# Where a fused attention and mixture kernel adds up, inverts and turns its softmax rows: moving three steps in VectorE's order of work

## The reference

```python
# stage 1: linear attention, then an MLP with a residual
q_s = softmax(q, axis=-1); k_s = softmax(k, axis=tokens)
x = q_s @ (k_s.T @ v)                                # per head
x = x + relu(normalize(x) * g_ln @ w_ch1) @ w_ch2    # normalize over 512 values
# stage 2: four causal attention experts, of which each token keeps the best two
logits = x @ w_gate                       # the two largest of 4, softmaxed, are the gates
for e in range(4):
    q, k, v = x @ wq[e], x @ wk[e], x @ wv[e]
    a = softmax(causal(q @ k.T / 8))
    out += gate_e * (a @ v @ wo[e])
```

## Time and profile before

| | |
|---|---|
| profiled execution, its own time | 1260.09 us |
| span of its trace | 1258.3 us |
| PE busy | 1229.3 us (98%) |
| DVE busy | 667.9 us (53%) |
| ACT busy | 379.5 us (30%) |
| POOL busy | 224.2 us (18%) |
| mean granted TensorE clock | 0.993 |
| stage 2 | about 891 to 1258 us, 42.4 us a batch |

### The profile page before, as it was taken

How to read it: one execution, slowest core, us unless ns; L and a number is a source line. 1 busy time by engine, 2 the same in 40 slices (tenths; PEclk the granted TensorE clock), 3 DMA queues, 4 the chain that set the end, 5 groups by cost and what they waited for, 6 DMA issues and landing times.

```text
span 1258.3 us, 19440 instructions
## 1 busy us (share of the span) xinstructions
PE 1229.3 (98%) x7136; PEld 1018.5 (81%) x7136; DVE 667.9 (53%) x1750; ACT 379.5 (30%) x858; POOL 224.2 (18%) x252
## 2 busy tenths in 40 slices
PE   8989999999999999999999999999989999999988
PEld 7878888888888888888888888888877787878876
DVE  5685365365365365365365313311576666666562
ACT  4462131131131131131131101121334445454445
POOL 3532000000000000000000000001474356445322
PEclk9999999999999999999999999999989999999999
DMA  8741540550550450460460230240356867786742
GB/s 186 177 103 48 133 72 11 129 79 9 126 85 6 120 94 5 117 98 5 108 106 5 68 67 16 67 104 1 89 158 167 242 188 216 207 239 189 183 132 76
DMA packets 344736, 133.06 MB, mean 106 GB/s; under 512 B 240960, under 2 KB 329024, under 8 KB 344640
## 3 DMA queue, kind: packets, MB, share of 16 engines
q1 hardware_dynamic: 296400, 108.85, 36.2%
q10 hardware_dynamic: 48240, 22.94, 7.2%
HBM read 72.10 MB, written 42.86 MB: 91 GB/s over the span
## 4 chain that ended last, share of the span: by engine, by line
PE 80%; DVE 9%; DMA 3%; ACT 3%; SPq 3%; issue 2%; ACTq 0%; POOL 0%; DVEq 0%; POOLq 0%
PE hb L1434 31%; PE yb L1522 30%; PE sc L1434 10%; PE pa L1451 3%; DMA turned<-px 2%; PE ob L1678 2%; DVE px L1358 2%; SPq L672 1%; DVE prob L1376 1%; PE pa L1442 1%; ACT prob L978 1%; PE tb L1644 1%; PE sc L1644 1%; SPq L531 1%; DVE k_lo L1295 1%
## 5 line engine op out<-in xcount | busy, mean ns | idle before, releaser
L1228 DVE SCALAR_TENSOR_TENSOR hid_lo<-hb,hid_hi 128x512 fp32r<-128x512 f32 x144 | 99.4, 690 | 383.1 <-ACT hid_hi L868 383.1
L868 ACT ACTIVATE hid_hi<-hb 128x512 fp32r<-128x512 f32 x144 | 85.8, 597 | 614.7 <-PE hb L1434 614.7
L1522 PE MATMUL yb<-hid_hi,w_hi 128*128 128x512 f32 x576 | 226.5, 393 | 2.4 <-DVE hid_lo L1228 2.4
L1434 PE MATMUL hb<-xn_hi,w_hi 128*128 128x512 f32 (+1 forms) x580 | 228.1, 393 | 0.0
L1434 PE MATMUL hb<-xn_lo,w_hi 128*128 128x512 f32 (+1 forms) x580 | 225.1, 388 | 0.0
L1434 PE MATMUL hb<-xn_hi,w_lo 128*128 128x512 f32 (+1 forms) x580 | 225.0, 388 | 0.0
L1522 PE MATMUL yb<-hid_hi,w_lo 128*128 128x512 f32 x576 | 224.3, 389 | 0.0
L1522 PE MATMUL yb<-hid_lo,w_hi 128*128 128x512 f32 x576 | 224.1, 389 | 0.0
L1434 PEld LDWEIGHTS hb<-xn_hi,w_hi 128*128 128x128 f32 x580 | 108.9, 188 | 25.6 <-issue 2.2
L1522 PEld LDWEIGHTS yb<-hid_hi,w_hi 128*128 128x128 f32 x576 | 108.1, 188 | 25.0 <-issue 2.8
L1434 PEld LDWEIGHTS hb<-xn_hi,w_lo 128*128 128x128 f32 x580 | 108.9, 188 | 22.8
(11 more groups left out here) (221 smaller groups left out, 1857.1 us busy)
## 6 DMA issues: line engine op xcount, KB each, us to landing
qx<-in_q_dram SPq DMA_DIRECT2D x32, 288.0 KB, 5.5
ksb<-in_k_dram SPq DMA_DIRECT2D x8, 1024.0 KB, 5.7
vsb<-in_v_dram SPq DMA_DIRECT2D x32, 256.0 KB, 4.8
stage<-in_moe_w_ch_dram SPq DMA_DIRECT2D x16, 512.0 KB, 4.1
xn_lo<-ksb SPq DMA_DIRECT2D x128, 64.0 KB, 2.0
y_scratch<-ysb SPq DMA_DIRECT2D x32, 256.0 KB, 2.9
ysb<-xsb SPq DMA_DIRECT2D x128, 64.0 KB, 2.1
out_dram<-osb SPq DMA_DIRECT2D x32, 256.0 KB, 4.1
```

The costliest lines, as they stand in the source:

```text
L868: act.activation(HID[f % 2][0][:], hb[f % 2][:], ACT.Relu).then_inc(sems["hhi_a"], 1)
L1228: dve.scalar_tensor_tensor(out=lo[:], in0=hb[f % 2][:], scalar=0.0, in1=plain(hi[:]), op0=ALU.max, op1=ALU.subtract).then_inc(sems["hlo_v" ...
L1434: ins = pe.matmul(dst, l, r, start=(n == 0), stop=(n == len(terms) - 1))
L1522: ins = pe.matmul(yb[j][:], l, r, start=(f == 0 and m == 0 and not first), stop=(f == FT - 1 and m == 2), skip_group_check=True)
```

## The change

On DVE `over_sum` is cut in two: the addition now comes one step later, ahead of that step's low part (`fill_lo`), the inversion behind it. `turn_blocks` moves from lag 3 to lag 4, SP's write from 3 to 4, ACT's `land` from 6 to 7. PE's steps, POOL's and the tables don't change. Between the stages, the tail's cast and low part move from ahead of V1 (ACT) and V2 (DVE) to just ahead of M2's.

```diff
@@ sync (SP), batch @@
-                    for k, shift in twos_at(n, 3, first, last):
+                    for k, shift in twos_at(n, 4, first, last):
                         if not (last and shift == 0):
                             write_turned(st, shift, k)
@@ scalar (ACT), batch @@
-                    for k, shift in twos_at(n, 6, first, last):
+                    for k, shift in twos_at(n, 7, first, last):
                         if not (last and shift == 0):
                             land(st, shift, k)
@@ scalar (ACT), between the stages @@
-                if i == 1:
+                if f == ("M", 2):
                     need(act, "y_v", (PAIRS, 0), KT)
                     act.copy(Y[0][0][:, :, CW:S], ysb[:, 0, :, 0:TAIL]).then_inc(y0hi_a, 1)
@@ vector (DVE) @@
-            def over_sum(st, shift, k, last):
+            def over_sum(st, shift, k, last, part):
                 us = units_of(k, last and shift == 0)
                 x = rrec[:, :, us[0] : us[-1] + 1]
-                need2(dve, "exp_a", st, shift, us[-1] + 1)
-                dve.tensor_scalar(x[:, 0], rsum[:, us[0] : us[-1] + 1], EPS_SUM, None, ALU.add).then_inc(sems["rrec_v"], 1)
-                need2(dve, "rrec_v", st, shift, 2 * k + 1)
-                dve.reciprocal(x[:, 1], x[:, 0]).then_inc(sems["rrec_v"], 1)
+                if part == 0:
+                    need2(dve, "exp_a", st, shift, us[-1] + 1)
+                    ins = dve.tensor_scalar(x[:, 0], rsum[:, us[0] : us[-1] + 1], EPS_SUM, None, ALU.add)
+                else:
+                    need2(dve, "rrec_v", st, shift, 2 * k + 1)
+                    ins = dve.reciprocal(x[:, 1], x[:, 0])
+                ins.then_inc(sems["rrec_v"], 1)
@@ vector (DVE), batch @@
                     if n < UNITS and second(n, last):
                         masked(st, n, first, last)
+                    for k, shift in twos_at(n, 2, first, last):
+                        over_sum(st, shift, k, last, 0)
                     if fill_at(n - 1, first, last):
                         f, shift = fill_at(n - 1, first, last)
                         fill_lo(st, shift, f, bank(n - 1))
+                    for k, shift in twos_at(n, 2, first, last):
+                        over_sum(st, shift, k, last, 1)
                     if n < UNITS and not second(n, last):
                         masked(st, n, first, last)
                     for w, shift in weighed(n - 1, first, last):
                         sums_lo(st, shift, w, last and shift == 0)
-                    for k, shift in twos_at(n, 1, first, last):
-                        over_sum(st, shift, k, last)
-                    for k, shift in twos_at(n, 3, first, last):
+                    for k, shift in twos_at(n, 4, first, last):
                         if not (last and shift == 0):
                             turn_blocks(st, shift, k)
@@ vector (DVE), between the stages @@
-                if i == 2:
+                if f == ("M", 2):
                     dve.wait_ge(y0hi_a, KT + 1)
                     dve.tensor_tensor(Y[0][1][:, :, CW:S], ysb[:, 0, :, 0:TAIL], plain(Y[0][0][:, :, CW:S]), ALU.subtract).then_inc(y0lo_v, 1)
```

## The result

The changed kernel took 1281.35 us (median of 4 runs, 1279.8 to 1283.27). The kernel before took 1261.52 in the same comparison. The ratio is 1.0152, 95% interval 1.0119 to 1.0185, so the change costs about 20 us. Forecast were 1273, range 1254 to 1293, slower with 0.67. The profiled execution took 1284.22 us, its span is 24.1 us longer than that of before.

A forecast was written before the change was run, and what follows sets the result against it. PE, busy 98% of the span, was taken as the bound. Terms -2.4 + 15.6 + 0 - 1.0 + 1.4 = +13.6 us gave a span of 1271.9, plus 1.8 makes 1273.7, stated as 1273; range 1254 to 1293.

The forecast's parts named there:

- six steady waits go: Steady batches, 950 to 1210 us: PE's six waits, for low parts and masks among others, all vanish, -2.4 us.
- (0, 1), six batches: PE's product needing group 4, six steady batches: later turn leaves 7.9 us, so a new wait of 1.0 us each.
- (1, 1), six batches: PE's product needing group 9, six steady batches: later turn leaves 7.1 us, so a new wait of 1.6 us each.
- tail: Between the stages: PE stands 1.5 us ahead of M2, hidden in a later 1.95 us `k_lo` wait; price 0.
- first batch: First batch: product (0, 1) 1.7 us later, the 2.65 us `k_lo` wait behind it absorbed; -1.0 us.
- last batch: Batch 6, group 9's product at 1221.40: same chain through memory, +1.4 us; the wait at 1216.51 may go.
- 8.9 us from turn to PE: Groups 4 and 9, turn's end through write and return to PE's product: between 8.2 and 9.7 us, taken as 8.9.
- rival 2: PE's clock falls to half for a stretch behind new waits of about 1.6 us: 1283, up to 1302 us; chance 0.22.
- Short chain: Steady batches: turn to product takes only 8.2 us, so the loss is small, +4.5, 1264.6 us; chance 0.13.
- faster: Turn to `pt` takes under 7.1 us, no new waits, first batch gives time back: -9.9, 1250 us; chance 0.14.
- nothing: PE's old waits go but others of that size come, so the order gives nothing: 1260 us; chance 0.07.
- DMA price by the Trainium skill: Writes and returns through memory: time mostly the memory's acknowledgement, tenfold when busy; would put every chain at the upper end.

The follow-up runs named there:

- small output stores: Changed kernel with each output store of batches 0 to 6 writing one row, 2 KB in place of 256 KB: 1272.4 us, ratio 1.0096 to the kernel before.
- product a step later: Changed kernel with PE's weighted product (0, 1) one step later, at step 0 of the next batch: 1277.0 us, ratio 1.0126 to the kernel before.

## Why the prediction was right, and where it was off

The direction and the mechanism were right: the turn and its write a step later make PE stand at the weighted products. The lags alone show the loss, the split and the tail alone nothing. The size was 14 for 20 us (24 in the profile). It would have been farther off had two errors at the two products not cancelled, which is luck. Its terms, in the order of the sum:

| term | forecast | in the profile after |
|---|---|---|
| six steady waits go | -2.4 | -2.4, all gone |
| (0, 1), six batches | 6 x 1.0 | 11.7 |
| (1, 1), six batches | 6 x 1.6 | 3.4 |
| (1, 0) | none | 3.3 |
| tail | 0 | absorbed alone; see below |
| first batch | -1.0 | PE 3.3 later at its product (1, 1) |
| last batch | +1.4 | +0.8: 1.2 at (1, 1), 1.3 more for POOL's scaling, 0.3 for a mask, the 2.0 of 1216.51 gone |
| TensorE's clock | none in the forecast | +4.3 behind the first batch |

The clock's term is (1 - clock) x 3 us summed over the stretches of stage 2: 13.6 us, 9.3 before, 6.8 of each in the first batch. Behind it 3.4 us are lost at two steady waits, where nothing was lost before, and 3.4 in the last batch, where it was 2.5. The waits for POOL's scaling, before and after:

```profile
PE tb L1656 <- POOL prob L808: 1.1, 2, 0.7
PE tb L1661 <- POOL prob L808: 2.4, 2, 1.3
```

The 0.5 us that PE waited at the first batch's (1, 1) stand in two rows. Counted once, the terms add up to 23.9 of the 24.1 us.

*The chain was one number for two places.* I took 8.9 us from turn to PE at both products. The sum of the two, 15.6, came out nearly right (15.1) because the errors cancelled. At (0, 1) it was 8.7 to 10.6 in the six batches, 9.5 on average and 9.9 in the one followed above. At (1, 1) it was 7.6 to 9.0, 8.2 on average: in the batch of 1063.09 the turn ended at 1055.35 and PE went on 7.7 us later without a wait. The room was mis-sized too. Chain less wait is some 7.6 us at both products, where I had 7.9 at (0, 1) and 7.1 to 7.4 at (1, 1). The code could have told it: output products stand at steps 10 to 14, so of the two only group 4 is written among output stores. "SP gets group 4's write behind one more output store: nothing either" was the wrong sentence: with small output stores the waits at (0, 1) are 6.6 us less.

*"For groups 9 and 4 it is more: the turn now stands behind `ot_lo`"* was right about the step and wrong as the cause to mend. With the turn ahead of `ot_lo` the (0, 1) waits stayed at 11.4 us, because the write then stood behind a store and landed beside the 512 KB return. Both orders had to be mended.

*The return's step.* I moved the return with the rest and priced only the groups that end a half. Returns one step later leave (1, 0), two steps behind its last return, too little time for a 256 KB DMA of 5.2 us: 3.3 us, shown by the kernel that changes nothing else.

*The tail.* Alone it is absorbed, as forecast. In the whole change the M2 wait was 2.26 in place of 1.34 us:

```profile
902.39 0.39 PE L1439 MATMUL sc<-y_hi,wqk_hi 128*128 128x320 f32 x1 [2.26 <-DVE y_lo L1423]
```

DVE, then GpSimd:

```profile
900.92 1.33 DVE L1423 TENSOR_TENSOR y_lo<-ysb,y_hi 128x256 fp32r<-128x256 f32 x1
```

```profile
900.82 1.15 POOL L784 TENSOR_TENSOR y_hi<-y_in,ones 128x576 fp32r<-128x576 f32 x1 [9.60 <-DMA y_in<-y_scratch]
```

The same instruction took 0.42 us before. Here GpSimd had started 0.10 us ahead of it, and it took 1.33. In the tail-only kernel it started 0.03 us ahead of GpSimd's and took 0.41:

```profile
900.14 0.41 DVE L1418 TENSOR_TENSOR y_lo<-ysb,y_hi 128x256 fp32r<-128x256 f32 x1
```

```profile
900.17 1.40 POOL L784 TENSOR_TENSOR y_hi<-y_in,ones 128x576 fp32r<-128x576 f32 x1 [9.73 <-DMA y_in<-y_scratch]
```

Then GpSimd's took 1.40 in place of 1.15. The Trainium skill (SBUF — State Buffer, "SBUF: two separate sides") says that VectorE with two SBUF inputs and GpSimd share a port pair, which the one that starts first keeps for its whole instruction. Both pairs of rows agree. I had seen the mark of it in `gcmp` of 910.20 and did not ask whether the moved `y_lo` would fall into it. It is a race of 0.1 us, and the traces show both outcomes: of the nine kernels with the moved tail three waited 1.34 us ahead of M2 (the tail alone, turn ahead of `ot_lo`, product a step later), the other six 2.1 to 2.3. In the whole change this was not absorbed. Behind the next wait PE went on at 919.52, at the same place before at 917.37: 2.2 us later, of which 0.5 had come about ahead of M2. So most of the 3.3 us in the table was there already. How much of it is the tail's stays open, since the split alone is 1.5 us late at this place and the tail alone 0.2.

*The first batch.* I expected the `k_lo` wait of 2.65 to make room for a later product (0, 1). It went, but the product waited 3.84 us (1.19 before) and carried it all.

*The clock, rival 2.* It fell, behind 2.34 and 2.45 us of waiting but not behind 1.92 or 2.17, and once more in the last batch behind four waits of 0.3 to 1.3 us: about 4 us more than before for the whole, not 10 to 29. Of the Trainium skill's rule that TensorE's recent activity sets one of two rates (TensorE: Matmul & The Clock Gate, Part 1) the forecast said that scattered waits may well pass; most did, the longest didn't.

*Short chain, faster, nothing:* out. *DMA price by the Trainium skill:* the write was slower when the queues were full, 4.0 against 2.3 us, which is not tenfold. The page's tenfold is for the memory's part alone, which no run here shows by itself.

## What to carry to other kernels

When a step of a chain through DRAM is moved, price every consumer of it with its own chain: what else its queue has just issued, and which large transfer on the other queue will now start beside it. A small write that started 2 us ahead of a large return mostly landed much sooner than one that started with it, and the order inside a step (transpose, write, then store) can be worth most of what the step costs: it gave back 15 of 20 us here. And a wait of one in-order engine for a DMA must be followed to all that stands behind it, since it decides which engine shows the loss.

## What was not expected of the hardware

- An 80 KB write in four DMAs landed in 2.3 us when issued 1.85 us ahead of a 512 KB return on the other queue, in 4.0 us when issued 0.12 us ahead of it; but 3.7 us were seen at a distance of 1.8 too. A 320 KB return took 3.7 us where it was issued 5.8 us behind the 512 KB one, 4.4 where 1.7 and 6.3 where 1.4 us behind it.
- The VectorE instruction of 0.42 us took 1.33 us when GpSimd's began 0.10 us ahead of it.
- PE's waits of 1.92 and 2.17 us between busy stretches left the granted clock at 1.00; waits of 2.34 and 2.45 were followed by 3 us at 0.56 and 0.52. In the last batch waits of 1.13, 1.26, 0.30 and 1.22 us within 8 us came with nearly 7 us at 0.50.
- Two kernels with nearly the same waits at their weighted products differed by 5 us, as much as TensorE's clock cost less in one of them (8.2 against 13.6 us).
